# A fused attention, Fourier mixing, MLP and expert kernel: MLP weight chunks in order of use, one spectrum step later, twenty of them in the first tile

## The reference

```python
# 1: windowed attention, 8 heads of 64, softmax over at most 128 earlier keys
x = attention(q, k, v)                       # (4, 576, 512)
# 2: Fourier mixing, then an MLP with a residual
X = np.fft.fft(np.fft.fft(x, axis=1), axis=2)
u = x + np.real(X)
un = (u - mean(u)) / sqrt(var(u) + 1e-6)
x = u + np.maximum(un @ w_ch1, 0.0) @ w_ch2  # w_ch1 (512, 2048), w_ch2 (2048, 512)
# 3: a mixture of 8 experts (512 to 1024 to 512), one expert a token, with a sticky gate
```

## Time and profile before

| | |
|---|---|
| median of 3 runs | 987.25 us (985.24 to 988.3) |
| time of the profiled execution | 985.19 us |
| its span in the trace | 983.4 us |
| PE busy | 923.3 us (94% of the span) |
| DVE, ACT, POOL busy | 457.1, 357.5, 284.2 us |

### The profile page before, as it was taken

The page is one execution under the profiler, slowest core; times in us unless marked ns, Lnnn a source line. Parts: engine busy times, 40 slices in busy tenths (PEclk is TensorE's granted clock), DMA queues, the critical chain, the costliest instruction groups (busy, mean ns, idle before and its releaser), DMA issues.

```text
span 983.4 us, 20128 instructions
## 1 busy us (share of the span) xinstructions
PE 923.3 (94%) x7739; PEld 584.8 (59%) x7740; DVE 457.1 (46%) x843; ACT 357.5 (36%) x475; POOL 284.2 (29%) x298
## 2 busy tenths in 40 slices
PE   5899998999999999999999999928999999999996
PEld 3566666456676767677767677614555555555552
DVE  4788887464523333333333343758973773000000
ACT  3677776353211212122121112012444444444442
POOL 2467766400111102020201000002443444333331
PEclk9999999899999999999999999968999999999998
DMA  8245542525201010110101102514763672111100
GB/s 284 82 149 160 165 141 64 162 84 160 65 23 44 22 43 29 35 43 21 43 21 43 43 0 74 171 36 122 252 202 124 220 223 80 43 42 49 50 13 1
DMA packets 55340, 89.21 MB, mean 91 GB/s; under 512 B 7140, under 2 KB 26035, under 8 KB 55165
## 3 DMA queue, kind: packets, MB, share of 16 engines
q1 hardware_dynamic: 49853, 72.56, 23.7%
q0 software_dynamic: 5440, 16.00, 5.3%
HBM read 71.19 MB, written 16.55 MB: 89 GB/s over the span
## 4 chain that ended last, share of the span: by engine, by line
PE 85%; DVE 8%; DMA 3%; issue 2%; ACT 1%; SPq 1%; POOL 0%; DVEq 0%; POOLq 0%; ACTq 0%
PE psum L803 19%; PE psum L820 19%; PE psum L979 13%; PE psum L955 13%; PE psum L598 4%; PE psum L742 3%; PE psum L754 2%; PE psum L968 2%; DVE m_mem L1251 2%; DVE arena L1279 2%; PE psum L943 1%; PE psum L764 1%; PE psum L619 1%; PE psum L653 1%; PE psum L672 1%
## 5 line engine op out<-in xcount | busy, mean ns | idle before, releaser
L803 PE MATMUL psum<-m_mem,arena 128*128 (+1 forms) x1728 | 198.8, 273 | 0.3 <-DVE arena L1511 0.3
L820 PE MATMUL psum<-arena,m_mem 128*128 128x512 f16 x864 | 195.3, 379 | 0.0
L803 PEld LDWEIGHTS psum<-m_mem,arena 128*128 128x128 f16 x1728 | 168.4, 98 | 26.0 <-DVE arena L1511 0.6
L820 PEld LDWEIGHTS psum<-arena,m_mem 128*128 128x128 f16 x864 | 84.6, 98 | 90.4
L955 PE MATMUL psum<-arena,m_mem 128*128 x600 | 135.2, 382 | 0.5 <-ACT m_mem L1184 0.5
L1119 ACT ACTIVATE m_mem<-psum 128x512 f16<-128x512 f32 x72 | 43.0, 597 | 250.1 <-PE psum L803 249.1
L979 PE MATMUL psum<-arena,m_mem 128*128 x600 | 133.6, 379 | 0.0
L955 PEld LDWEIGHTS psum<-arena,m_mem 128*128 128x128 f16 x600 | 58.2, 99 | 66.6 <-issue 2.8
L1419 DVE SCALAR_TENSOR_TENSOR m_mem<-psum,m_mem 128x512 f16<-128x512 f32 x72 | 49.7, 691 | 103.4 <-ACT m_mem L1119 102.6
L979 PEld LDWEIGHTS psum<-arena,m_mem 128*128 128x128 f16 x600 | 57.7, 98 | 65.4 <-issue 0.4
L1756 POOL TENSOR_TENSOR arena<-m_mem,arena 128x1024 f16<-128x1024 f32 x9 | 18.0, 1995 | 272.2 <-ACT arena L1134 227.2
(11 more groups left out here) (220 smaller groups left out, 1156.4 us busy)
## 6 DMA issues: line engine op xcount, KB each, us to landing
dimdft_sb<-in_exp_w SPq DMA_DIRECT2D x74, 256.0 KB, 3.2
wstage<-in_exp_w SPq DMA_DIRECT2D x54, 256.0 KB, 3.2
m_mem<-in_qk SPq DMA_DIRECT2D x16, 576.0 KB, 4.5
arena<-in_v SPq DMA_DIRECT2D x32, 160.0 KB, 4.3
x_rows<-m_mem SPq DMA_DIRECT2D x16, 320.0 KB, 3.3
x_rows<-arena SPq DMA_DIRECT2D x9, 512.0 KB, 2.8
wstage<-in_mlp_w SPq DMA_DIRECT2D x16, 256.0 KB, 3.2
arena<-in_mlp_w SPq DMA_DIRECT2D x16, 256.0 KB, 2.9
```

Source lines behind the costliest of these rows:

```text
L803: last = nc.tensor.matmul(psum[:, 2 + k % 4, (f % 2) * 2 * P:(f % 2 + 1) * 2 * P], w1_sb[:, sp_, c, f * P:(f + 1) * P], unT[:, bass.ds(t % ...
L820: last = nc.tensor.matmul(psum[:, 6 + q, :], hT[:, k % 4, sp_, at:at + P], w2_sb[:, mp, f, :], start=f == 0 and sp_ == 0 and mp == 0, stop ...
```

## The change

The loads and conversions take the chunks in another order and at other places. `W_ORDER` lists the chunks as the first tile uses them: the first two column groups of `w_ch1` (8 chunks), the first four chunks of `w_ch2`, the third group, four chunks of `w_ch2`, the fourth group, the last eight chunks of `w_ch2`. From here on "chunk n" of the changed kernel is the n-th in that order.

Four chunks are converted ahead of the spectrum steps as before. Chunks 4 to 11 follow steps 1 to 8, so chunk 4 comes one step later, and steps 0 and 9 to 15 have none. The other twenty are converted in the first tile: 3, 3, 3, 3, 4, 4 after `hidden` 0 to 5. PE's waits on `w_split` ask for what each block needs. On SP three loads (chunks 12 to 14) now end the run of early loads, chunk 15 takes the place of chunk 23, and chunks 16 to 31 are behind the tables that chunks 24 to 31 were behind. The wait of the lo part for `x_split` and `table_made` moves from old chunk 15 to new chunk 8, the first whose lo part lies in the memory that is in use until then.

```diff
+PER_F = FF // CH
+W_UP = [[c * PER_F + g for c in range(DC)] for g in range(PER_F)]
+W_DOWN = [DC * PER_F + f for f in range(FF // P)]
+W_ORDER = W_UP[0] + W_UP[1] + W_DOWN[0:4] + W_UP[2] + W_DOWN[4:8] + W_UP[3] + W_DOWN[8:]
+W_SPEC = 4
+W_DFT = 8
+W_TILE0 = [3, 3, 3, 3, 4, 4, 0, 0]
+def w_count(chunks):
+    return max(W_ORDER.index(n) for n in chunks) + 1
+def w_tile0(k):
+    at = W_SPEC + W_DFT + sum(W_TILE0[0:k])
+    return range(at, at + W_TILE0[k])
...
-                sp.dma_start(w_staging[n % WRING], mlp_w[n]).then_inc(w_loaded[n % WRING], 16)
+                sp.dma_start(w_staging[n % WRING], mlp_w[W_ORDER[n]]).then_inc(w_loaded[n % WRING], 16)
...
-            W_TOP = W_SPEC + DC * B
+            W_TOP = W_SPEC + W_DFT
...
-                if first and k == 0:
-                    pe.wait_ge(w_split, DC * FF // CH)
+                if first and k % 2 == 0:
+                    pe.wait_ge(w_split, w_count(W_UP[k // 2]))
...
-                    pe.wait_ge(w_split, DC * FF // CH + 2 * k + 2)
+                    pe.wait_ge(w_split, w_count(W_DOWN[2 * k:2 * k + 2]))
...
# spectrum_hi, and the same in spectrum_lo
-                    w_hi_of(W_SPEC + DC * b + c)
+                    if 0 < DC * b + c <= W_DFT:
+                        w_hi_of(W_SPEC + DC * b + c - 1)
...
# ACT and DVE in the first tile, after hidden k
-                    for n in range(W_SPEC + DC * B + 2 * k, min(WCH, W_SPEC + DC * B + 2 * k + 2)):
+                    for n in w_tile0(k):
...
-                if n == W_FREE:
+                at = W_ORDER[n]
+                if at >= W_FREE and n == min(W_ORDER.index(i) for i in range(W_FREE, WCH)):
                     dve.wait_ge(x_split, PAIRS)
                     dve.wait_ge(table_made, 2)
```

More of the change, by code:

```diff
@@ L64 @@
 ECH = EW // CH
-assert WCH == 2 * DC * B and ECH == 2 * (MT - 1)
+assert ECH == 2 * (MT - 1)
+PER_F = FF // CH
+W_UP = [[c * PER_F + g for c in range(DC)] for g in range(PER_F)]
+W_DOWN = [DC * PER_F + f for f in range(FF // P)]
+W_ORDER = W_UP[0] + W_UP[1] + W_DOWN[0:4] + W_UP[2] + W_DOWN[4:8] + W_UP[3] + W_DOWN[8:]
+assert sorted(W_ORDER) == list(range(WCH))
+W_SPEC = 4
+W_DFT = 8
+W_TILE0 = [3, 3, 3, 3, 4, 4, 0, 0]
+assert W_SPEC + W_DFT + sum(W_TILE0) == WCH
+def w_count(chunks):
[3 more added lines that the diff above has]
+    return range(at, at + W_TILE0[k])
 NSLOT = 4
@@ L201, in fused_kernel @@
         W_FREE = (xsh_at - w_at - W_WORDS // 2) // CH
-        W_SPEC = 4
         rows_at = w_at + W_WORDS
@@ L1080, in w_hi_of @@
                 act.wait_ge(w_loaded[n % WRING], 16 * (n // WRING + 1))
-                nc.scalar.activation(wparts[:, 0, n * CH:(n + 1) * CH], w_staging[n % WRING], ACT.Copy, scale=WS)\
+                at = W_ORDER[n]
+                nc.scalar.activation(wparts[:, 0, at * CH:(at + 1) * CH], w_staging[n % WRING], ACT.Copy, scale=WS)\
                     .then_inc(w_hi, 1)
@@ L1297, in w_lo_of @@
                 dve.wait_ge(w_hi, n + 1)
-                if n == W_FREE:
+                at = W_ORDER[n]
+                if at >= W_FREE and n == min(W_ORDER.index(i) for i in range(W_FREE, WCH)):
                     dve.wait_ge(x_split, PAIRS)
                     dve.wait_ge(table_made, 2)
-                nc.vector.scalar_tensor_tensor(out=wparts[:, 1, n * CH:(n + 1) * CH], in0=w_staging[n % WRING], scalar=WS,
-                                               in1=wparts[:, 0, n * CH:(n + 1) * CH], op0=ALU.mult,
+                nc.vector.scalar_tensor_tensor(out=wparts[:, 1, at * CH:(at + 1) * CH], in0=w_staging[n % WRING], scalar=WS,
+                                               in1=wparts[:, 0, at * CH:(at + 1) * CH], op0=ALU.mult,
                                                op1=ALU.subtract).then_inc(w_split, 1)
@@ L1360, in spectrum_lo @@
                             w_lo_of(n)
-                    w_lo_of(W_SPEC + DC * b + c)
+                    if 0 < DC * b + c <= W_DFT:
+                        w_lo_of(W_SPEC + DC * b + c - 1)
             spectrum_lo(0, (0,))
```

## The result

The changed kernel takes 979.71 us in the median of 10 runs (978.42 to 983.21); the kernel before, run beside it, 986.51 us (10 runs, 983.8 to 989.47). The ratio is 0.9935, 95% interval 0.9918 to 0.9951: 6.4 us less, between 4.8 and 8.1. In a second comparison ("after_again") it was 0.9949, 0.9931 to 0.9967, or 5.0 us. The forecast was 5.05 us less, and 982.2 us for the median. Runs of one kernel differ by about 5 us here, and the interval is as wide for that reason.

What follows compares the result with a forecast made beforehand. PE, busy 94% of the span, was taken as the bound. Wait 2.15 plus clock 3.0 minus first tile 0.1 gave 5.05 us, subtracted from the 987.25 us median: 982.2 us, range 979.5 to 986 us.

Steps and rivals of the forecast that it cites:

- The stall goes: At spectrum step 3, PE's wait of 2.15 us for step 1's lo part disappears.
- The wait for chunk 4: ACT waits for it after step 1's hi part, hidden from PE with 0.3 us margin at step 4.
- The spare of 0.6 us at step 3: DVE ends step 1's lo part at 176.0, and PE is free for step 3 at 176.67.
- this very collision: First tile: DVE conversions meeting POOL's work on the shared port; two meetings ahead of `normalise_u` would stall PE 0.4 us.
- Rival B: The wait only moves one step on, to step 4, if chunk 4 lands late: about 984 to 985 us, chance 0.10.
- The clock: Spectrum steps 3 to 5: without the standstill the granted clock doesn't fall, and 54 matmuls gain 3.0 us.
- the two terms: At spectrum steps 3 to 5: the removed wait, 2.15 us, and the lowered clock behind it, 3.0 us.
- Fewer conversions in steps 9 to 15: Steps 0 and 9 to 15 lose a conversion each on ACT and DVE, which had time there: gain 0.
- The wait for `x_split`: It comes at spectrum step 5 instead of step 11: cost 0.
- The first tile: With 20 chunks instead of 12, `normalise_u` ends 1.2 us later, 0.8 us margin before `transpose_un(1)`; 0.1 us charged.
- rival C: First tile becomes the bound through late chunk loads: 5.4 us loss at 5.1 us landing, 990.3 us at 6.5; chance 0.05.
- Rival A: The 2.15 us go, but the lowered clock stays or falls elsewhere, such as the second `edge`: 985.2 us, chance 0.14.

Runs made afterwards that it cites:

- after_again: The changed kernel, unchanged, run a second time beside the kernel before: 981.05 us, ratio 0.9949.
- e1: Kernel before, chunk order kept, each spectrum-step chunk converted one step later, 13 chunks in the first tile instead of 12: 980.79 us, ratio 0.9935.
- e2: Changed kernel with its eight chunks after spectrum steps 0 to 7, so chunk 4 follows step 0 again: 984.58 us, ratio 0.9980.
- e3: Kernel before plus nine matmuls whose result nobody reads, on PE between spectrum steps 2 and 3: 983.35 us, ratio 0.9959.
- e4b: Changed kernel with the second edge begun ahead of the last lo part, repeat run: 978.12 us, ratio 0.9919.
- e5: Changed kernel with 4 chunks in the spectrum steps instead of 8, and 24 in the first tile: 986.95 us, ratio 1.0015.
- e6: Changed kernel with no chunks in the spectrum steps and 28 in the first tile: 990.06 us, ratio 1.0057.
- before_again: The kernel before, unchanged, run once more for a second trace: 986.44 us, one run.
- e2b: Repeat of the changed kernel with chunk 4 after spectrum step 0 again: 984.91 us, ratio 0.9998.
- e4: Changed kernel whose second edge does its first 18 of 24 matmuls before waiting for the last lo part: 979.23 us, ratio 0.9921.

## Why the prediction was right, point by point

1. **The stall goes: right.** 2.15 us forecast; e1 and e2 show that the one step does it, e3 gives 2.4 us for it, and the traces without the step have 2.15 to 2.60.
2. **The wait for chunk 4 is hidden, with 0.3 us to spare at step 4: right in place, and the margin was 0.4 us** (the lo part of step 2 ends at 177.42, step 4 starts at 169.97 + 54 x 0.146 = 177.85).
3. **The spare of 0.6 us at step 3 was wrong.** I took 0.24 us for the small instructions, from a trace in which DVE did them when POOL was not in their way. One step earlier they fall beside POOL's work. In six of the eight traces that have the change's order of steps and these instructions at their place they take 1.2 us, and the spare is just used up. In the other two (e4b, e5) they take 1.9 us, since the second meets POOL's 1.39 us instruction instead of the 0.64 us one, and PE waits 1.2 us. The prediction weighed this very collision, but for the first tile. The Trainium skill ("SBUF — State Buffer", section "Who interferes with whom") has the rule: a VectorE instruction with two SBUF inputs, or one in a two-port mode, which its list says a `tensor_scalar` can enter, and a GpSimd instruction that reads SBUF hold a shared port in turns, the one behind blocked until the other has ended. The trace agrees: each of the two ends within 0.05 us of the POOL instruction; which mode the TENSOR_SCALAR ran in, no run shows. In the first tile, for which I had priced it at up to 0.4 us, no conversion ahead of `normalise_u` shows a meeting (0.68 to 0.69 us alone, 1.28 to 1.36 for two). Rival B so came true in part, at step 3 and for another reason than the landing of chunk 4.
4. **The clock: right in kind, and the size partly luck, since it came from one trace.** 3.0 us forecast from 10.91 us; the other three traces with a bare standstill have 9.45 to 9.51 us, which is 1.5 to 1.6 us over 7.92. So the two terms together are worth 5.1 us against the first trace of before and 3.9 to 4.1 us against the other three. Prediction and check against the first trace agree so well because both use its longer fall.
5. **Fewer conversions in steps 9 to 15: right to 0.2 us** where I said 0. The wait for `x_split`, now at step 5, cost nothing, as forecast: the trace after has no wait of PE in steps 1 to 15.
6. **The first tile: right.** `moments` and `normalise_u` 1.2 us later (249.19 + 5.10 = 254.29 against 253.10), margin 0.79 us for 0.8 forecast, 416.00 us for the MLP before and after. e5 and e6 show that it was close: four chunks more cost 3.6 us there. The clock's part of rival C's price came with the standstill of 4.37 us (e6) and not with that of 3.42 us (e5).
7. **Rival A**, the clock falling elsewhere, came true in the profiled run, in the second `edge`. But nothing here says that it is the change's doing: among the ten traces with that standstill of 1.8 us the clock fell in five (before_again, after, e1, e2b, e3) and held in five (before, after_again, e2, e5, e6).
8. **Median and profiled run.** I subtracted from the median, and the result is 2.5 us lower than the forecast of 982.2, only 0.2 us above the lower end of the stated range. 0.7 us of this is the starting point: the kernel before has 986.51 us in ten runs and had 987.25 in three. The rest is a gain of 6.8 us between the medians for 5.05 forecast. In the second comparison it would have been 985.48 - 5.05 = 980.4 for 981.05 measured.

   What no trace shows, how much low clock there is in all the other runs, can be estimated, since every run lists its span and its mean granted clock. Span times clock is the time at full clock throughout; the rest of the span is put down to low clock, wherever it lies, also where PE stands still and it costs nothing. The means of all runs then part so:

   | run | spans shorter by | of this at full clock | low clock |
   |---|---|---|---|
   | e1 | 6.2 | 2.5 | 3.7 |
   | after_again | 4.8 | 2.3 | 2.5 |
   | e3 | 3.2 | -0.3 | 3.5 |
   | e2 | 2.1 | 0.3 | 1.8 |
   | e2b | 0.1 | -0.1 | 0.2 |

   The standard errors are 0.4 to 0.7 us in the third column and 0.6 to 1.3 us in the last. The third column fits the traces: the wait (2.15 to 2.60 us) goes in e1 and after_again and stays in e3, where only the clock is held. The last gives 2.5 to 3.7 us for the clock, near the 3.0 forecast but not sharper than about 1 us. It also holds most of what differs between e2 and e2b, where the program is the same. Compared in the same way, e5's spans are 6.1 us longer than after_again's, 3.9 at full clock and 2.2 low clock.

## What to carry to other kernels

In an engine's queue an instruction that waits for a late transfer holds everything behind it: a prefetch step belongs behind the work that another engine is waiting for, even if it is needed first. A standstill of TensorE of some 2 us can cost more than itself, since the matmuls behind it may run at the lower clock (four of four traces at 2.15 to 2.60 us, five of ten at 1.8). Filling it with idle matmuls (e3) gets back the clock and not the wait; starting the part of the next work that is ready (e4) gets back both. A duration taken from a trace holds for its place there: moved beside GpSimd's work, a VectorE instruction of 0.2 us took 1.3.

## What the runs showed of the hardware that I had not expected

Standstills of the same length in the same kernel are followed by a lower clock in one execution and not in the next: 1.8 us ahead of the second `edge`, five of ten; 3.7 us inside the first expert block, ahead of its transposes (L968, later L985), eleven of fourteen. There the granted clock stays 1.00 in after, e1 and e6 and falls to 0.50 for a while in the others, before among them, which makes the experts' 308.3 to 308.9 or 309.9 to 310.9 us. A standstill of 3.42 us in e5 was followed by no fall. The start of step 1 lies between 169.97 and 173.84 us, with nothing changed ahead of it. Each of the two moves a time by 1.6 to 3.9 us, with a gain of 5 us to be measured. The first, second and third runs of one kernel (e4) so gave ratios from 0.9919 to 0.9950.
